# A gated scan and an ELU feed-forward on one core: where the tensors begin in SBUF, shifted to multiples of 512 bytes

## The chip, the cores and the metric

The kernel runs on one core of a Trainium2 chip. The metric is the device time of one launch in microseconds (us). Before the change three runs took 1008.64 us (median), between 1008.42 and 1009.03.

## What is computed

A gated recurrence over 6080 time steps, for 2 sequences of 256 channels, and then a feed-forward layer with an ELU on each of its 12160 outputs:

```python
sig = 1.0 / (1.0 + np.exp(-f_logit))                 # (2, 6080, 256)
f = lower_bound + (1.0 - lower_bound) * sig
for t in range(S):
    h = f[:, t] * h + (1.0 - f[:, t]) * x[:, t]
    y[:, t] = h
u = y.reshape(12160, 256) @ w_in                     # w_in (256, 2048)
g = np.where(u > 0.0, u, np.exp(np.minimum(u, 0.0)) - 1.0)
out = g @ w_out                                      # w_out (2048, 256)
```

## The kernel before, in words

**Layout.** Channels lie on the 128 partitions (256 channels are 2 halves), time runs along the free dimension. A block `j` is 512 steps of both sequences; there are 12 blocks, and the last is 448 steps wide (`width`). The 2048 hidden units are 16 units of 128, taken in 8 pairs `q`.

**Precision.** Every operand of a product is split into a high part of type fp32r and a rest, its low part, of the same type (4 bytes per element each). One product is three matmuls, each with a weight load of 128x128 of its own: high weights by high data, high weights by low data, low weights by high data (`product`, L828 to L837; `second`, L839 to L866). The streamed operand is called the moving one here, the loaded one the weights.

**First product.** For a pair `q` the four tiles C11, C12, C22, C21 (2 units by 2 sequences) are formed out of seven products P1 to P7 in place of eight, from sums of the data (`a_hi`, `a_lo`, `a4_hi`, `a4_lo`) and sums of the weights (`w_in_hi`, `w_in_lo`). They go to PSUM banks `h`; ScalarE copies one bank (`fork`, L434), VectorE makes two additions (`add_u4`, L678; `add_c22`, L686). Block 0 has no summed weights yet and uses plain products (`first_products`, L920 to L942, and `first_product`, L944 to L958), with the low weights in `w_plain_low`.

**ELU.** For each tile ScalarE makes Relu(-h) (L442) and Exp (L448) in `e`, VectorE combines them (L692), ScalarE rounds the result to `g_hi` (L456) and GpSimd subtracts for `g_lo` (L315). `g_hi` and `g_lo` are rings of 8 tiles of 2048 bytes.

**Second product.** For each tile two halves of three matmuls (L860, L861, L862) with moving operand `g_hi`, `g_lo`, `g_hi` add up in PSUM `acc`. They are issued one pair, or two for C21, behind the tile's own products (`whole` of the tensor engine, L868 to L913), so a pair is 45 matmuls: 21 with a moving operand `a...` and 24 with `g...`. A block is 360 matmuls; there are 10 whole blocks of this kind, after block 0 and ahead of the short one.

**Order.** Each engine has its program written out by hand: VectorE's spare work (opening the gates, weighing, the scans, copying `acc` out) stands in fixed places of the pair loop (`spare`, `whole`), and semaphores alone tie the engines. The scan, its loads and the splits of block `j + 1` run in block `j`.

**Memory.** All tensors are allocated one after another in a partition (`sb`, L71); four pairs of names share one room (`alloc_sbuf_tensor_at`). The first free byte at the start, rounded up to 32, is 16512, which is 32 x 512 + 128. All large tensors have a size that is a multiple of 512 bytes. Between `a4_lo` and `e` stand four small ones (`carry`, `bound`, `slope`, `offset`; 16, 8, 8 and 8 bytes, each begun at a multiple of 32), which take 128 bytes in all. A weight operand is 128 columns x 4 bytes = 512 bytes long and begins at its tensor's start plus a multiple of 512; a moving operand is 2048 bytes and begins at its tensor's start plus a multiple of 2048.

```python
        weights_at = -(-nc.sbuf_base // 32) * 32
        sb("weights_room", [P, PAIRS * (in_cols + out_cols) + BATCH * HALVES * TILE])
        nc.tensor.matmul(bank[:, 0:w], hi, a_h[:, 0:w], start=start, stop=False,
        nc.tensor.matmul(bank, hi, g_hi[:, t % RING, 0:w], start=opens, stop=False)
```

Of the kernel before, what the change touches and what calls it, by code (L numbers as in the profile page):

```python
# [8 lines left out]
F32R = mybir.dt.float32r  # L9

P = 128
# [7 lines left out]
TILE = 512  # L19
BLOCKS = -(-SEQ // TILE)  # L20
SHORT = SEQ - (BLOCKS - 1) * TILE
TILES = 4
RING = 8
# [44 lines left out]
def gated_scan_elu_ffn(nc, forget_logit, value, lower_bound, w_in, w_out, out):  # L68
    ctx = ExitStack()
    with ctx:  # L70
        def sb(name, shape, dt=F32):  # L71
            return ctx.enter_context(nc.sbuf_tensor(name, shape, dt))
# [3 lines left out]


        in_cols, out_cols = PRODUCTS * P, 2 * D
        weights_at = -(-nc.sbuf_base // 32) * 32
        sb("weights_room", [P, PAIRS * (in_cols + out_cols) + BATCH * HALVES * TILE])  # L80
        w_in_raw = nc.alloc_sbuf_tensor_at("w_in_raw", [P, PAIRS, PRODUCTS, P], F32, offset=weights_at)
# [21 lines left out]
            w_plain_low.append(nc.alloc_sbuf_tensor_at(f"w_plain_lo{p}", [P, 4, P], F32R, offset=at))  # L103
        a4_hi = sb("a4_hi", [P, TILE], F32R)
        a4_lo = sb("a4_lo", [P, TILE], F32R)
        carry = sb("carry", [P, BATCH, HALVES, 1])
        bound = sb("bound", [P, HALVES])
        slope = sb("slope", [P, HALVES])
        offset = sb("offset", [P, HALVES])

        e = sb("e", [P, TILES, TILE])
        p5 = sb("p5", [P, TILE])
        g_hi = sb("g_hi", [P, RING, TILE], F32R)
        g_lo = sb("g_lo", [P, RING, TILE], F32R)


        h = ctx.enter_context(nc.psum_tensor("h", [P, 4, TILE], F32))
# [894 lines left out]
```

## Time and profile before

| | |
|---|---|
| median of three runs | 1008.64 us |
| the profiled execution | 1008.46 us |
| its span, first to last instruction | 1006.6 us |
| TensorE busy, share of the span | 100% |
| ScalarE, VectorE, GpSimd busy | 79%, 73%, 63% |
| granted TensorE clock | 1.00 of full (2.4 GHz) |

The profile's page gives each engine's busy time, the chain of waits that ended last and the costliest groups of instructions. PE is TensorE's matmul, PEld its weight load, DVE VectorE, ACT ScalarE, POOL GpSimd. A matmul's recorded duration is modelled and overlaps the next one; what a matmul costs in a full stream is the distance between two starts, called its pitch here. Profile times are counted from the span's start. The execution's own time lies 1.86 us over its span.

### The profile page before, as it was taken

Reading aid. Unit: us, or ns where it says so; the run is one execution under the profiler, and the core shown is the slowest. Engines: PE = TensorE matmul, PEld = TensorE weight load, DVE = VectorE, ACT = ScalarE, POOL = GpSimd, SP = SyncE. Lnnn points to the kernel's source line nnn. Section 1 sums busy time; section 2 is a strip of 40 time slices with the busy share of each in tenths; the row PEclk is TensorE's granted clock in tenths of the full one; section 3 lists DMA queues with packets and bytes.
Section 4 is the critical chain, followed back from the end, with each engine's and each line's share of the span. In section 5 each row is a group of like instructions: output and inputs, shape, how many; then the busy total and the mean of one; then the engine's idle time right before and its main releaser. Section 6 shows DMA issues by size and latency. Waiting matters only on the chain.

```text
span 1006.6 us, 15352 instructions
## 1 busy us (share of the span) xinstructions
PE 1001.7 (100%) x4362; PEld 817.3 (81%) x4362; DVE 731.0 (73%) x915; ACT 791.6 (79%) x1425; POOL 631.4 (63%) x474
## 2 busy tenths in 40 slices
PE   9999999999999999999999999999999999999998
PEld 6888888888888888888888888888888888888997
DVE  6995876886786697588679668758867957875544
ACT  7987878777877877877787787787778778778775
POOL 2586887567557557656755855765675575566454
PEclk9999999999999999999999999999999999999999
DMA  7112002101201100210210120011021011000001
GB/s 272 63 32 63 33 1 74 53 1 52 73 0 42 52 31 0 73 52 0 63 63 0 42 63 21 18 55 52 0 64 61 0 46 64 5 0 9 36 1 37
DMA packets 23211, 41.88 MB, mean 42 GB/s; under 512 B 2704, under 2 KB 4240, under 8 KB 23184
## 3 DMA queue, kind: packets, MB, share of 16 engines
q1 hardware_dynamic: 22752, 41.04, 12.6%
q10 hardware_dynamic: 432, 0.53, 0.2%
q8 instruction: 12, 0.20, 0.1%
q14 instruction: 15, 0.12, 0.0%
HBM read 29.10 MB, written 12.45 MB: 41 GB/s over the span
## 4 chain that ended last, share of the span: by engine, by line
PE 99%; DMA 1%; ACT 0%; SPq 0%; DVE 0%; issue 0%
PE acc L862 18%; PE acc L860 18%; PE acc L861 17%; PE h L834 14%; PE h L832 14%; PE h L836 14%; PE h L956 1%; PE h L957 1%; PE h L955 1%; DMA w_in_raw<-w_in 1%; PE h L927 0%; PE h L936 0%; PE acc L927 0%; PE acc L956 0%; PE acc L957 0%; PE acc L955 0%
## 5 line engine op out<-in xcount | busy, mean ns | idle before, releaser
L315 POOL TENSOR_TENSOR g_lo<-e,g_hi 128x512 fp32r<-128x512 f32 (+1 forms) x384 | 518.6, 1359 | 369.5 <-ACT g_hi L456 369.3
L442 ACT ACTIVATE e<-h 128x512 f32<-128x512 f32 (+1 forms) x380 | 225.6, 594 | 166.2 <-PE h L836 135.0
L692 DVE SCALAR_TENSOR_TENSOR e<-e,h 128x512 f32<-128x512 f32 (+1 forms) x380 | 257.1, 677 | 77.3 <-ACT e L448 77.1
L862 PE MATMUL acc<-g_hi,w_out_lo 128*128 128x512 f32 (+1 forms) x768 | 301.9, 393 | 0.0
L860 PE MATMUL acc<-g_hi,w_out_hi 128*128 128x512 f32 (+1 forms) x768 | 301.0, 392 | 0.0
L861 PE MATMUL acc<-g_lo,w_out_hi 128*128 128x512 f32 (+1 forms) x768 | 299.7, 390 | 0.0
L456 ACT CAST g_hi<-e 128x512 fp32r<-128x512 f32 (+1 forms) x384 | 232.2, 605 | 20.7 <-DVE e L692 20.7
L448 ACT ACTIVATE e<-e 128x512 f32<-128x512 f32 (+1 forms) x384 | 241.6, 629 | 8.4
L834 PE MATMUL h<-a_lo,w_in_hi 128*128 128x512 f32 (+1 forms) x616 | 240.8, 391 | 0.0
L832 PE MATMUL h<-a_hi,w_in_hi 128*128 128x512 f32 (+1 forms) x616 | 240.0, 390 | 0.0
L836 PE MATMUL h<-a_hi,w_in_lo 128*128 128x512 f32 (+1 forms) x616 | 238.7, 388 | 0.0
L862 PEld LDWEIGHTS acc<-g_hi,w_out_lo 128*128 128x128 f32 x768 | 144.0, 187 | 32.6
L861 PEld LDWEIGHTS acc<-g_lo,w_out_hi 128*128 128x128 f32 x768 | 144.2, 188 | 31.6
L860 PEld LDWEIGHTS acc<-g_hi,w_out_hi 128*128 128x128 f32 x768 | 144.2, 188 | 30.1
L832 PEld LDWEIGHTS h<-a_hi,w_in_hi 128*128 128x128 f32 x616 | 115.7, 188 | 26.9
L834 PEld LDWEIGHTS h<-a_lo,w_in_hi 128*128 128x128 f32 x616 | 115.6, 188 | 25.0
L836 PEld LDWEIGHTS h<-a_hi,w_in_lo 128*128 128x128 f32 x616 | 115.7, 188 | 24.4
L686 DVE TENSOR_TENSOR h<-p,h 128x512 f32<-128x512 f32 (+1 forms) x88 | 60.5, 687 | 74.5 <-PE h L836 74.5
L601 DVE TENSOR_TENSOR_SCAN x<-gate,carry,x 128x512 f32<-128x512 f32 x48 | 104.2, 2171 | 0.1
L671 DVE COPY p<-h 128x512 f32<-128x512 f32 (+1 forms) x88 | 59.2, 673 | 57.8 <-PE h L836 57.8
L678 DVE TENSOR_TENSOR h<-p,h 128x512 f32<-128x512 f32 (+1 forms) x88 | 60.2, 684 | 39.1 <-PE h L836 38.3
L593 DVE SCALAR_TENSOR_TENSOR x<-gate,x 128x512 f32<-128x512 f32 x48 | 57.3, 1194 | 1.6 <-ACT gate L405 1.3
(72 smaller groups left out, 569.7 us busy)
## 6 DMA issues: line engine op xcount, KB each, us to landing
out<-out_sb SPq DMA_DIRECT2D x44, 256.0 KB, 2.0
gate<-forget_logit SPq DMA_DIRECT2D x43, 256.0 KB, 2.7
x<-value SPq DMA_DIRECT2D x43, 256.0 KB, 2.7
w_in_raw<-w_in SPq DMA_DIRECT2D x8, 256.0 KB, 6.5
w_out_raw<-w_out SPq DMA_DIRECT2D x8, 256.0 KB, 7.4
x<-value SPq DMA_DIRECT2D x4, 224.0 KB, 2.5
gate<-forget_logit SPq DMA_DIRECT2D x4, 224.0 KB, 2.5
out<-out_sb SPq DMA_DIRECT2D x4, 224.0 KB, 2.0
```

The lines of the kernel that those rows point to most:

```text
L315: nc.gpsimd.tensor_tensor(g_lo[:, t % RING, 0:w], e[:, t % TILES, 0:w], g_hi[:, t % RING, 0:w].bitcast(F32), ALU.subtract).then_inc(g_lo_r ...
L442: nc.scalar.activation(e[:, i, 0:w], bank_of(j, t)[:, 0:w], ACT.Relu, scale=-1.0).then_inc(r_ready, 1)
L448: nc.scalar.activation(e[:, t % TILES, 0:w], e[:, t % TILES, 0:w], ACT.Exp, scale=-1.0).then_inc(e_ready, 1)
L456: nc.scalar.copy(g_hi[:, t % RING, 0:w], e[:, t % TILES, 0:w]).then_inc(g_hi_ready, 1)
L601: nc.vector.tensor_tensor_scan(x[:, b, i, 0:w], gate[:, b, i, 0:w], x[:, b, i, 0:w], carry[:, b, i], ALU.mult, ALU.subtract).then_inc(scan ...
L692: nc.vector.scalar_tensor_tensor(e[:, t % TILES, 0:w], e[:, t % TILES, 0:w], -1.0, bank_of(j, t)[:, 0:w], ALU.add, ALU.max).then_inc(g_rea ...
L832: nc.tensor.matmul(bank[:, 0:w], hi, a_h[:, 0:w], start=start, stop=False, skip_group_check=True)
L834: nc.tensor.matmul(bank[:, 0:w], hi, a_l[:, 0:w], start=False, stop=False, skip_group_check=True)
L836: return nc.tensor.matmul(bank[:, 0:w], lo, a_h[:, 0:w], start=False, stop=True, skip_group_check=True)
L860: nc.tensor.matmul(bank, hi, g_hi[:, t % RING, 0:w], start=opens, stop=False)
L861: nc.tensor.matmul(bank, hi, g_lo[:, t % RING, 0:w], start=False, stop=False)
L862: done = nc.tensor.matmul(bank, lo, g_hi[:, t % RING, 0:w], start=False, stop=closes)
```

## The change

Ahead of the weights a tensor `room_before` that nothing reads or writes fills up the space to the next multiple of 512 (384 bytes). The four small tensors move from between `a4_lo` and `e` to the end. No instruction is added, removed or reordered on any engine; the addresses in them are all that differs.

```diff
@@ -76,6 +76,9 @@
         in_cols, out_cols = PRODUCTS * P, 2 * D
+
+        base = -(-nc.sbuf_base // 32) * 32
+        sb("room_before", [P, -base % 512], mybir.dt.uint8)
         weights_at = -(-nc.sbuf_base // 32) * 32
         sb("weights_room", [P, PAIRS * (in_cols + out_cols) + BATCH * HALVES * TILE])
@@ -103,15 +106,14 @@
         a4_hi = sb("a4_hi", [P, TILE], F32R)
         a4_lo = sb("a4_lo", [P, TILE], F32R)
+        e = sb("e", [P, TILES, TILE])
+        p5 = sb("p5", [P, TILE])
+        g_hi = sb("g_hi", [P, RING, TILE], F32R)
+        g_lo = sb("g_lo", [P, RING, TILE], F32R)
         carry = sb("carry", [P, BATCH, HALVES, 1])
         bound = sb("bound", [P, HALVES])
         slope = sb("slope", [P, HALVES])
         offset = sb("offset", [P, HALVES])
-
-        e = sb("e", [P, TILES, TILE])
-        p5 = sb("p5", [P, TILE])
-        g_hi = sb("g_hi", [P, RING, TILE], F32R)
-        g_lo = sb("g_lo", [P, RING, TILE], F32R)
```

The starts, in bytes of a partition, and what is left of them over a multiple of 512, as the allocations give them:

| tensor | before | over 512 | after | over 512 |
|---|---|---|---|---|
| `w_in_raw`, `w_in_lo` | 16512 | 128 | 16896 | 0 |
| `w_out_raw`, `w_out_lo` | 45184 | 128 | 45568 | 0 |
| `out_sb`, `w_plain_lo0` to `3` | 61568 | 128 | 61952 | 0 |
| `w_in_hi` | 69760 | 128 | 70144 | 0 |
| `w_out_hi` | 98432 | 128 | 98816 | 0 |
| `gate`, `x` | 114816, 123008 | 128 | 115200, 123392 | 0 |
| `a_hi`, `a_lo` | 131200, 155776 | 128 | 131584, 156160 | 0 |
| `a4_hi`, `a4_lo` | 180352, 182400 | 128 | 180736, 182784 | 0 |
| `e`, `p5` | 184576, 192768 | 256 | 184832, 193024 | 0 |
| `g_hi`, `g_lo` | 194816, 211200 | 256 | 195072, 211456 | 0 |
| `carry` and the other three | 184448 to 184552 | | 227840 to 227944 | |

So before, weights and `a...` lie 128 bytes over a multiple of 512, and `e`, `p5` and `g...` 256 bytes over one.

## Rows read from the trace of the kernel before

**Rows 1.** The page: span, and busy time of each engine

```profile
span 1006.6 us, 15352 instructions
...
PE 1001.7 (100%) x4362; PEld 817.3 (81%) x4362; DVE 731.0 (73%) x915; ACT 791.6 (79%) x1425; POOL 631.4 (63%) x474
```

**Rows 2.** The waits, TensorE alone: who for whom, us in total, times, longest

```profile
PE h L963 <- POOL e L372: 1.3, 1, 1.3
PE h L927 <- ACT a_hi L417: 0.5, 1, 0.5
```

**Rows 3.** Stretches, TensorE alone, one whole block each: length, busy time (count), clock

```profile
340.31:423.55 83.24, 83.24 (x362) 1.00 0.12 38
506.79:590.03 83.24, 83.24 (x362) 1.00 0.12 38
```

**Rows 4.** Timeline of TensorE in block 0: start us, us, instruction

```profile
11.80 0.39 PE L933 MATMUL h<-a_lo,w_in_hi 128*128 128x512 f32 x1
...
17.25 0.39 PE L955 MATMUL h<-a_hi,w_in_hi 128*128 128x512 f32 x1
...
18.61 0.40 PE L860 MATMUL acc<-g_hi,w_out_hi 128*128 128x512 f32 x1
...
20.00 0.39 PE L955 MATMUL h<-a_hi,w_in_hi 128*128 128x512 f32 x1
...
21.38 0.40 PE L860 MATMUL acc<-g_hi,w_out_hi 128*128 128x512 f32 x1
```

**Rows 5.** Timeline of TensorE in a whole block, around its third pair

```profile
451.98 0.40 PE L860 MATMUL acc<-g_hi,w_out_hi 128*128 128x512 f32 x1
452.21 0.39 PE L861 MATMUL acc<-g_lo,w_out_hi 128*128 128x512 f32 x1
452.43 0.40 PE L862 MATMUL acc<-g_hi,w_out_lo 128*128 128x512 f32 x1
452.67 0.39 PE L860 MATMUL acc<-g_hi,w_out_hi 128*128 128x512 f32 x1
452.90 0.40 PE L861 MATMUL acc<-g_lo,w_out_hi 128*128 128x512 f32 x1
453.14 0.39 PE L862 MATMUL acc<-g_hi,w_out_lo 128*128 128x512 f32 x1
...
454.07 0.39 PE L832 MATMUL h<-a_hi,w_in_hi 128*128 128x512 f32 x1
```

**Rows 6.** Timeline of TensorE at the end of its warm-up, bf16 matmuls on `e`

```profile
7.07 1.03 PE L963 MATMUL h<-e 128*128 128x512 bf16 x4
...
7.50 0.59 PE L963 MATMUL h<-e 128*128 128x512 bf16 x2
```

**Rows 7.** Timeline of TensorE in the last block, 448 columns wide

```profile
984.37 0.36 PE L832 MATMUL h<-a_hi,w_in_hi 128*128 128x448 f32 x1
...
985.60 0.36 PE L860 MATMUL acc<-g_hi,w_out_hi 128*128 128x448 f32 x1
...
1000.06 0.36 PE L862 MATMUL acc<-g_hi,w_out_lo 128*128 128x448 f32 x1
...
1002.91 0.37 PE L861 MATMUL acc<-g_lo,w_out_hi 128*128 128x448 f32 x1
```

**Rows 8.** Timeline of VectorE up to the addition that P4 of rows 5 waits for

```profile
441.87 0.70 DVE L686 TENSOR_TENSOR h<-p,h 128x512 f32<-128x512 f32 x1 [0.47 <-PE h L836]
...
443.89 0.69 DVE L692 SCALAR_TENSOR_TENSOR e<-e,h 128x512 f32<-128x512 f32 x1 [0.74 <-ACT e L448]
444.50 2.32 DVE L601 TENSOR_TENSOR_SCAN x<-gate,carry,x 128x512 f32<-128x512 f32 x1
...
450.00 1.79 DVE L593 SCALAR_TENSOR_TENSOR x<-gate,x 128x512 f32<-128x512 f32 x1
451.71 1.52 DVE L586 TENSOR_SCALAR gate<-gate,slope,offset 128x512 f32<-128x512 f32 x1
453.15 0.68 DVE L686 TENSOR_TENSOR h<-p,h 128x512 f32<-128x512 f32 x1
```

**Rows 9.** Groups of instructions on ScalarE: busy, mean ns of one, idle before

```profile
L456 ACT CAST g_hi<-e 128x512 fp32r<-128x512 f32 (+1 forms) x384 | 232.2, 605 | 20.7 <-DVE e L692 20.7
...
L427 ACT CAST a_hi<-x 128x512 fp32r<-128x512 f32 (+1 forms) x33 | 20.4, 617 | 0.0
```

**Rows 10.** The chain of waits in order of time, its beginning: start us, us, what

```profile
1.65 5.74 DMA w_in_raw<-w_in
7.41 0.62 ACT w_in_hi L464
8.03 0.53 ACT a_hi L417
8.60 1.25 PE h L927 x4
```

## The prediction

> **What bounds the kernel now.** Read the page's busy times first [rows 1]: TensorE is busy for 1001.7 of 1006.6 us. That alone doesn't say that it works at its best, since a matmul's end is modelled, so the second view is its waits [rows 2]: 1.3 us for its first operand and 0.5 us before the first real product, and nothing after. From 8.6 us to the end TensorE never waits for anyone. The third view is the stretches [rows 3]: two whole blocks far apart take 83.24 us each for 360 matmuls (the two more in the count reach over an edge), 231.2 ns a matmul. The clock is granted in full, so 512 columns at 2.4 GHz would be 213.3 ns, and 17.9 ns of each pitch is something else. It repeats to the hundredth of a microsecond from block to block, while the other engines' work around it differs. So the kernel is a row of 4362 pitches, and the question is what an address does to a pitch.
>
> The timeline answers part of it. In block 0, from 11.80 to 18.61 us, 30 matmuls have a moving operand `a...` only [rows 4]: 6.81 / 30 = 227.0 ns each. Then groups of six with `g...` alternate with six with `a...`: 18.61 to 20.00 is 1.39 us, 20.00 to 21.38 is 1.38 us, so 231.7 and 230.0 ns. In a whole block's run of nine with `g...` the distances go 0.23, 0.22, 0.24, 0.23, 0.24 and so on [rows 5], and 454.07 - 451.98 = 2.09 us is 232.2 ns each; leave out the first two and it is 1.64 / 7 = 234 ns. So with `g...` as moving operand a matmul comes to cost about 7 ns more than with `a...`, and the first few `a...` after a run of `g...` still pay part of it, which is why the mean is 231.2 and not the mean of 227 and 234 over the kinds alone.
>
> What differs between the two kinds? Not the columns, the type, the weight's size or the order high, low, high. Not PSUM: in the stretch of 30 the banks of both `h` and `acc` are written (`FIRST_BANK`), and they average the 227 all the same. Not which weight: their starts step by 512 bytes, and the pitch follows neither high nor low; it alternates by two where the operands change by three [rows 5]. What is left is that `a...` begins 128 bytes over a multiple of 512, as the weights do, and `g...` 256 over one, or 128 bytes apart from the weights. Since the load of the next weights runs beside the streaming of the present operand, and the pitch alternates and has an aftermath, I take it that the two reads of TensorE meet each other in SBUF, and that their distance within 512 bytes sets how often. After the change this distance is 0 everywhere, as it is for `a...` now.
>
> **The change part by part.**
>
> *The distance between `g...` and the weights goes from 128 to 0 bytes.* Every 512-column matmul then has the pitch of the stretch of 30. I use 226.7 ns, 0.3 under the quotient of those rows, as they include the tail of a start-up; either value is within their rounding (6.81 us to a hundredth, over 30). A whole block becomes 360 x 0.2267 = 81.61 us in place of 83.24, saving 1.63; ten of them save 16.3 us. Block 0 has 25 periods of twelve matmuls, each 2.77 us now [rows 4] and 12 x 0.2267 = 2.72 after: 25 x 0.05 = 1.2 us; its last 12 matmuls with `g...` give 12 x 0.007 = 0.1 us. In the last block the pitch is 2.85 / 14 = 203.6 ns with `g...` and 1.23 / 6 = 205 ns with `a...` [rows 7], alike, so I take nothing there but for the 30 matmuls of the block before it that lag into it: 0.15 us. Sum: 16.3 + 1.2 + 0.1 + 0.15 = 17.75 us.
>
> *The common offset goes from 128 to 0.* The trace has no operand at 0. By my reading only the distance counts and this is worth nothing. The bounds from rows: at best the matmul falls to the 216 ns of the warmed-up bf16 matmuls (four take 1.03 us and the last two of them 0.59, so a pitch is 0.44 / 2 = 0.22, a little under in finer time) [rows 6], at worst it goes to 234 ns. I take 226.7, since that row is nearest in everything but the common offset; the ends are rivals below.
>
> *What is late next.* With TensorE 1.9% faster, the place with least room is in the third pair of each block: VectorE works without a pause from 444.50 to 453.83 us [rows 8] (the end of its addition at L686, 453.15 + 0.68), and TensorE's P4 at 454.07 waits for that addition [rows 5]. The room is 0.24 us. VectorE's run begins behind an Exp (443.89) that hangs on the same addition one pair earlier, which started at 441.87 as soon as TensorE let it [rows 8]. From there to this P4 are 12.2 us, 53 matmuls, so TensorE will come earlier by 53 x 4.5 ns = 0.24 us, the whole room. With a semaphore's way P4 then waits about 0.05 us, once a block: 0.5 us in all. Behind the waiting matmul stands all of TensorE's queue, so this is on the path. If VectorE's operations were faster through the alignment there would be nothing; if its shared work with GpSimd fell worse by 0.1 us, another 1 us. I take 0.5, with 0 and 1.5 as ends.
>
> *The other engines' operands.* ScalarE's rounding takes 605 ns from `e` to `g_hi`, both 256 over, and 617 ns from `x` to `a_hi`, both 128 over [rows 9], means that mix some narrow tiles in. So these engines hardly see the offset; 2% either way, hidden behind TensorE. At the start the first weights' transfer of 5.74 us leads to the first product [rows 10]. Its rows of 2048 bytes now land on multiples of 512. Nothing in the trace shows a price; a tenth of the transfer, 0.6 us, either way bounds it. I take 0.
>
> *The four small tensors and the padding.* No one waits for where they lie, and the padding isn't touched: nothing.
>
> The sum goes against the profiled execution's 1008.46 us, 0.18 under the median: 1008.46 - 17.75 + 0.5 = 991.2. This case's own range is 988.5 to 993.5.
>
> A rule speaks against all of this. The Trainium skill, "SBUF — State Buffer", section "Who interferes with whom", gives TensorE two read ports, one for the moving operand and one for the weight load, and calls them independent. By that rule addresses would not matter and the sum would be 0. The trace doesn't settle it in words, but two kinds of matmul with different pitches under the same clock and the same shape are hard to fit to it. The page "TensorE: Matmul & The Clock Gate", section "Back-to-back issue gap", gives N / 2.4 + 2.5 ns for a warm matmul, 216 for 512 columns; the warm-up agrees [rows 6], the fp32r matmuls here do not.
>
> **The rivals.**
>
> *Aligned reads are cheaper still.* If a 512-byte weight that begins on a multiple of 512 spares something that one across a boundary pays, all pitches fall below 226.7. For it: 256 over costs more than 128 over, which continued gives about 220 at 0. Against: the alternation and the aftermath point at a meeting of two reads, not at a fee per boundary. Price: to the floor of 216 a block takes 77.8 us, 5.4 less; with block 0 about 59 us. P4's wait then grows to 53 x 15 ns - 0.24 = 0.6 us a block, 6 us in all, so 1008.5 - 59 + 6 = 955. Halfway, at 221, it is 1008.5 - 39 + 3 = 972. I write 965 for it.
>
> *The address isn't the cause.* `g...` is also the operand that ScalarE and GpSimd have just written and lies high in memory. Then nothing moves: 1008.5 us. For it: no pair of rows differs in the address alone. Against: the first matmuls of a run of `a...` after `g...` pay too, and whole blocks repeat to 0.01 us [rows 3] though the writers' timing within them varies. The two-port rule of the Trainium skill's page "SBUF — State Buffer" would lead to this case.
>
> *The common offset counts, the wrong way (the other side).* An operand at 0 might meet the load at its worst, since both reads then begin on the same boundary at once. The price is 234 ns for every matmul: a block takes 84.2 us, 1.0 more; with block 0 about 11.5 us, so 1020. It decides the sign as soon as the pitch at 0 is over 231.2 ns. For it: no row is at 0. Against: `a...` and the weights have the same offset already, and that is the cheaper kind.
>
> **How the numbers follow.** Chances: my forecast 0.55, cheaper still 0.20, no change 0.14, slower 0.11. A difference under 0.2%, 2 us, is about what a measurement of this kernel can't tell from none. So faster 0.75, same 0.14, slower 0.11. The range goes up to the case of no change, 1009, and leaves out the slower one; down it goes to 962, which leaves out the outer third of the cheaper case: 0.55 + 0.13 + 0.14 = 0.82 inside.
>
> **What would show it.** Right: whole blocks of 81.6 to 81.7 us in the stretches, all 512-column pitches at 226 to 227 with no alternation in a run of `g...`, the last block's 203.6 ns unchanged, and at most some small waits of TensorE for L686. Wrong: a pitch for `a...` off 227 (then the common offset counts), or `g...` still at 234 (then the address isn't the cause). If TensorE shows waits of more than 2 us in all, the gain is right and the cover was thinner than I read it.

## The result and the profile after

The changed kernel took 991.78 us (median of four runs, 991.58 to 992.14) against 1008.53 us of the kernel before beside it: a ratio of 0.9833, 95% interval 0.9816 to 0.9851. The forecast was 991.2 us. The profiled execution has a span of 989.8 us, 16.8 less than [rows 1].

The page's busy times and TensorE's waits:

```profile
span 989.8 us, 15352 instructions
PE 983.3 (99%) x4362; PEld 816.4 (82%) x4362; DVE 727.9 (74%) x915; ACT 791.4 (80%) x1425; POOL 631.7 (64%) x474
```

```profile
PE h L929 <- ACT a_hi L419: 1.3, 1, 1.3
PE h L965 <- POOL e L374: 1.3, 1, 1.3
PE h L957 <- issue: 0.6, 1, 0.6
```

The other engines do the same work in the same time to within 0.5%; their share rises only because the span is shorter. All of the difference is TensorE's. Its waits have a new row of 0.6 us, to which we come below. The wait ahead of the first product is 1.3 us where it was 0.5 [rows 2], but it costs nothing: the warm-up ended earlier in this execution, and the product itself began at 8.23 us in place of 8.60. Lines of the code lie two further down than before.

Here are two stretches of TensorE's, each from the start of P4 in the third pair of a block to the same start one block later, against 83.24 us in [rows 3]. TensorE is busy throughout, so the length between two such starts is what there is to read, here and in the stretches below, which run from a block's first matmul to the next block's:

```profile
283.18:364.86 81.68, 81.68 (x362) 1.00 0.12 39
446.54:528.22 81.68, 81.68 (x361) 1.00 0.12 39
```

TensorE's timeline in block 0 and at the third pair of a whole block, against [rows 4, 5]:

```profile
18.39 0.39 PE L862 MATMUL acc<-g_hi,w_out_hi 128*128 128x512 f32 x1
...
19.75 0.39 PE L957 MATMUL h<-a_hi,w_in_hi 128*128 128x512 f32 x1
...
21.11 0.39 PE L862 MATMUL acc<-g_hi,w_out_hi 128*128 128x512 f32 x1
```

```profile
444.50 0.39 PE L862 MATMUL acc<-g_hi,w_out_hi 128*128 128x512 f32 x1
444.73 0.39 PE L863 MATMUL acc<-g_lo,w_out_hi 128*128 128x512 f32 x1
444.95 0.39 PE L864 MATMUL acc<-g_hi,w_out_lo 128*128 128x512 f32 x1
...
446.54 0.45 PE L834 MATMUL h<-a_hi,w_in_hi 128*128 128x512 f32 x1
446.82 0.40 PE L836 MATMUL h<-a_lo,w_in_hi 128*128 128x512 f32 x1
```

Six matmuls with `g...` take 1.36 us and six with `a...` take 1.36 us: 226.7 ns each, where [rows 4] had 1.39 and 1.38. The run of nine takes 446.54 - 444.50 = 2.04 us, 226.7 ns each, where [rows 5] had 2.09, and the distances no longer alternate. Between the first two matmuls of P4, though, lie 0.28 us in place of 0.23. The addition that P4 waits for ends just ahead of it:

```profile
444.32 1.52 DVE L588 TENSOR_SCALAR gate<-gate,slope,offset 128x512 f32<-128x512 f32 x1
445.75 0.68 DVE L688 TENSOR_TENSOR h<-p,h 128x512 f32<-128x512 f32 x1
```

It ends at 446.43, 0.11 us before the recorded start of P4, where the room was 0.24 us before ([rows 8]). In nine of the ten whole blocks this distance is 0.28 to 0.29 us, and those blocks take 81.68 us; the first has none of it and takes 81.60, which is 360 x 226.67 ns.

The 0.6 us gap is in block 0. TensorE, and VectorE's ELU just before it:

```profile
76.64 0.39 PE L864 MATMUL acc<-g_hi,w_out_lo 128*128 128x512 f32 x1
77.64 0.47 PE L957 MATMUL h<-a_hi,w_in_hi 128*128 128x512 f32 x1 [0.61 <-issue]
```

```profile
76.85 0.69 DVE L694 SCALAR_TENSOR_TENSOR e<-e,h 128x512 f32<-128x512 f32 x1 [0.68 <-ACT e L450]
```

The matmul that starts at 77.64 belongs to tile 28. By `FIRST_BANK` it goes to bank 3, which tile 26 used last, and the ELU at 76.85 is tile 26's; it ends at 77.54. The "issue" of the trace is this wait for a PSUM bank. It costs 1.00 - 0.23 = 0.77 us, and the next distance is 0.08 longer too: 0.85 us in all.

### The profile page after: what moved, and what is told of

Its sections match the earlier page's. It is cut to its first block, busy times and chain, and to the rows that moved or that the text cites. A ratio compares the mean times of both kernels' runs of the same rounds, so it can differ in the third digit from the quotient of the medians.

```text
span 989.8 us, 15352 instructions
## 1 busy us (share of the span) xinstructions
PE 983.3 (99%) x4362; PEld 816.4 (82%) x4362; DVE 727.9 (74%) x915; ACT 791.4 (80%) x1425; POOL 631.7 (64%) x474
## 4 chain that ended last, share of the span: by engine, by line
PE 99%; DMA 1%; DVE 0%; issue 0%; ACTq 0%; ACT 0%
PE acc L864 17%; PE acc L862 17%; PE acc L863 17%; PE h L834 14%; PE h L836 14%; PE h L838 14%; PE h L957 1%; PE h L959 1%; PE h L958 1%; DMA x<-value 1%; PE h L938 0%; DVE x L603 0%; PE h L929 0%; PE acc L959 0%; PE acc L957 0%; PE acc L938 0%
## 5 line engine op out<-in xcount | busy, mean ns | idle before, releaser
L864 PE MATMUL acc<-g_hi,w_out_lo 128*128 128x512 f32 (+1 forms) x768 | 297.3, 387 | 0.0
L862 PE MATMUL acc<-g_hi,w_out_hi 128*128 128x512 f32 (+1 forms) x768 | 297.3, 387 | 0.0
L836 PE MATMUL h<-a_lo,w_in_hi 128*128 128x512 f32 (+1 forms) x616 | 238.4, 387 | 0.0
```

What stands on the lines that cost most here:

```text
L836: nc.tensor.matmul(bank[:, 0:w], hi, a_l[:, 0:w], start=False, stop=False, skip_group_check=True)
L864: done = nc.tensor.matmul(bank, lo, g_hi[:, t % RING, 0:w], start=False, stop=closes)
```

## The experiments

All times are medians beside runs of the kernel before on the same chip (1008.6 to 1008.8 us).

### Which part of the change does it

The change does two things: it moves everything to a multiple of 512, and it brings `e`, `p5` and `g...` to the same offset as the weights. These three runs take them apart.

Only the small tensors moved (the padding left out of the changed kernel):

```diff
-        base = -(-nc.sbuf_base // 32) * 32
-        sb("room_before", [P, -base % 512], mybir.dt.uint8)
```

> Only the four small tensors move to the end; no padding ahead of the weights, so weights, data and g all begin 128 bytes over a multiple of 512. Theory (the distance between the moving operand and the weights within 512 bytes sets the pitch): distance 0 everywhere as in the changed kernel, 991.8 us within 1 us, all 512-column pitches 226.7 ns. Rival (a start at a multiple of 512 is what is cheap): no better than the a... operands before, also 226.7 ns; if g... at 128 costs less or more than a..., the difference shows in its rows.

Measured: 992.12 us, ratio 0.9835 (0.9819 to 0.9852). Half of the diff, and none of the alignment, gives all of the gain.

Only the padding (the other half of the diff, the small tensors where they were):

```diff
+        base = -(-nc.sbuf_base // 32) * 32
+        sb("room_before", [P, -base % 512], mybir.dt.uint8)
         weights_at = -(-nc.sbuf_base // 32) * 32
```

> Only the padding ahead of the weights; the small tensors stay in the middle, so weights and a... begin at 0 and e, p5 and g... at 128 over a multiple of 512. Theory of the distance: as before the change, since g... is again 128 past the weights: 1008.5 us within 1.5, g pitches alternating 229 and 238 ns. Rival (the moving operand's own start over 512 counts: 128 is cheap, 256 dear, 0 at least as cheap): 991.8 us, all pitches 226.7 ns.

Measured: 1008.28 us, ratio 0.9996 (0.9987 to 1.0006): no difference from before. The weights and `a...` are at a multiple of 512 here, and the whole gain is missing. `g...` begins at 128 over a multiple, as `a...` did before the change at 227 ns, and costs what it cost at 256 over.

All at 256 over a multiple of 512:

```diff
-        sb("room_before", [P, -base % 512], mybir.dt.uint8)
+        sb("room_before", [P, (256 - base) % 512], mybir.dt.uint8)
```

> The changed kernel with all starts 256 bytes over a multiple of 512, padding and all. Theory of the distance: 991.8 us within 1 us, nothing changes. Rival (a moving operand that begins at 256 over is dear, whatever the weights do): every 512-column pitch goes to 234 ns, a block to 84.2 us, the kernel to about 1020 us.

Measured: 992.0 us, ratio 0.9835 (0.9818 to 0.9851). The offset that `g...` had when it was dear is cheap once the weights have it as well.

A whole block of each (the small tensors alone, the padding alone, all at 256), by the stretches:

```profile
335.58:417.27 81.69, 81.69 (x361) 1.00 0.12 39
```

```profile
340.41:423.64 83.23, 83.23 (x361) 1.00 0.12 38
```

```profile
335.04:416.73 81.69, 81.69 (x361) 1.00 0.12 39
```

So the moving operand's own start does not count, and neither does the common one. The distance between the two operands does.

### The price of each distance

Here TensorE runs extra stretches of 24 matmuls behind its last product, with no other computation beside most of them. They write PSUM banks that nothing reads any more. `CASES` gives the weights' start, the moving operand's start (in elements of 4 bytes) and the columns:

```diff
+CASES = ([(w, m, 512) for w in (0, 32, 64, 96) for m in (0, 32, 64, 96)]
+         + [(0, m, 512) for m in (1, 2, 4, 8, 16, 24, 40, 48, 80, 112)]
+         + [(16, 16, 512), (8, 16, 512)]
+         + [(0, 0, n) for n in (480, 448, 384, 256)] + [(0, 32, n) for n in (480, 448, 384, 256)])
...
+                weights = w_in_hi[:, :, :, :].rearrange("p a b c -> p (a b c)")[:, w_at:w_at + P]
+                moving = a_hi[:, :, :, :].rearrange("p a b c -> p (a b c)")[:, m_at:m_at + columns]
+                for k in range(24):
...
+                        nc.tensor.matmul(bank, weights, moving, start=k % 3 == 0, stop=k % 3 == 2)
```

> The changed kernel, and behind its last product 34 stretches of 24 matmuls that only write unused PSUM banks: weights at 0, 128, 256, 384 past a multiple of 512 by the moving operand at 0, 128, 256, 384 (16 stretches of 512 columns); weights at 0 with the moving operand at 4, 8, 16, 32, 64, 96, 160, 192, 320 and 448 bytes; both at 64; weights at 32 and moving at 64; then 480, 448, 384 and 256 columns, with the moving operand at 0 and again at 128. 34 x 24 x 0.23 = 180 us more or so in all. Theory of the distance: the four stretches with equal starts cost 226.7 ns each, the four with the moving operand 128 past the weights 233.4, and the other distances are constant along a diagonal too. Rival of the moving start: the price follows the moving operand's start alone. Rival of a fee per boundary crossed: only weights at 0 are cheapest. By width: if the weight load sets a floor, 448 and fewer columns stay near 203 ns.

TensorE's timeline, the rows for weights at 0 and then at 128 with the moving operand at 0, 128, 256, 384, and behind "..." weights at 0 with the moving operand at 4, 8, 16, 32 and 64 bytes (start us, us, instruction; two lines of code in turn, so that each stretch has its own row):

```profile
987.63 5.63 PE L997 MATMUL h<-a_hi,w_in_hi 128*128 128x512 f32 x24
993.09 5.75 PE L995 MATMUL h<-a_hi,w_in_hi 128*128 128x512 f32 x24
998.68 5.62 PE L997 MATMUL h<-a_hi,w_in_hi 128*128 128x512 f32 x24
1004.14 5.75 PE L995 MATMUL h<-a_hi,w_in_hi 128*128 128x512 f32 x24
1009.73 5.76 PE L997 MATMUL h<-a_hi,w_in_hi 128*128 128x512 f32 x24
1015.33 5.62 PE L995 MATMUL h<-a_hi,w_in_hi 128*128 128x512 f32 x24
1020.78 5.75 PE L997 MATMUL h<-a_hi,w_in_hi 128*128 128x512 f32 x24
1026.37 5.62 PE L995 MATMUL h<-a_hi,w_in_hi 128*128 128x512 f32 x24
...
1076.02 5.85 PE L997 MATMUL h<-a_hi,w_in_hi 128*128 128x512 f32 x24
1081.70 5.77 PE L995 MATMUL h<-a_hi,w_in_hi 128*128 128x512 f32 x24
1087.31 5.72 PE L997 MATMUL h<-a_hi,w_in_hi 128*128 128x512 f32 x24
1092.87 5.76 PE L995 MATMUL h<-a_hi,w_in_hi 128*128 128x512 f32 x24
1098.47 5.66 PE L997 MATMUL h<-a_hi,w_in_hi 128*128 128x512 f32 x24
```

Read the distance between starts over 24, or, leaving the first three of a stretch out, from the fourth start to the last over 20, as in this table:

| distance in bytes, moving less weights | pitch, ns |
|---|---|
| 0 (four offsets) | 226.7, the first stretch 227.2 |
| 0 (both operands at 64) | 227.8 |
| 256 (four) | 226.65 |
| 128 (four), 384 (four) | 233.3 |
| 64, 320 | 228.75 |
| 16 | 231.65 |
| 8, 32 (weights at 0, and at 32), 192, 448 | 233.3 |
| 96, 160 | 234.0, 234.35 |
| 4 | 236.7 |

The sixteen of the grid fall into two prices, strictly by distance, so the rival of the moving start and the fee per boundary both fall: weights at 128, 256 and 384 have a multiple of 512 inside them, weights at 0 have none, and at the same distance they cost the same. The 227.8 ns of the stretch with both operands at 64 is a slow beginning: its first nine matmul distances average 232 ns and the others 226.6; other stretches begin slowly too, for three to five matmuls. I had not expected that 0 and 256, and 128 and 384, are alike: the pattern repeats after 256 bytes, not 512. With 512 columns none of the distances tried is cheaper than 0. Fewer columns give no clear rule: with the operands 0 and 128 apart 480 columns take 216.7 and 217.65 ns, 448 take 206.4 and 203.55, 384 take 173.3 and 175.45, 256 take 119.7 and 118.7. So with 448 and 256 columns the distance of 128 is the cheaper one in these stretches. Nor do the stretches of 448 carry over to the kernel: in the last block of the changed kernel, with the distance 0 throughout, the 448-column matmuls take 202.6 ns on average and not 206.4. Why is open. A floor of 203 ns from the weight load, which the last block's nearly equal pitches [rows 7] suggested, does not exist, since 384 columns take 173.3.

### Does the price carry back into the kernel

A dear distance for every product, and a cheap one by another number. Both kernels leave room behind the weights, 32 bytes in one and 256 in the other:

```diff
+APART = 32
...
+        sb("apart", [P, APART], mybir.dt.uint8)
         gate = sb("gate", [P, BATCH, HALVES, TILE])
```

> The changed kernel with 32 bytes left free between the weights and everything behind them: every moving operand is then 32 bytes past the weights within 512 (233.35 ns in the probe, the same as 128). Theory: 6.7 ns more for each of the 360 matmuls, blocks of 84.0 in place of 81.68 us, block 0 about 2 us more less the 0.85 us wait that it has now, so 1015.5 us (1013 to 1018), slower than before the change. Rival (only multiples of 128 or 512 bytes matter, or the probe does not carry over to the kernel): 992 or 1008 us.

> The same with 256 bytes left free: weights at 0 and all data at 256 over a multiple of 512. Theory of a distance that repeats after 256 bytes, as the probe showed: 991.8 us within 1. Rival (it repeats after 512, the probe's stretches without other engines' work do not carry over): above 1000 us.

Measured with 32 bytes: 1018.05 us, ratio 1.0092 (1.0076 to 1.0107). With 256 bytes: 992.0 us, ratio 0.9835 (0.982 to 0.985). A whole block of each:

```profile
343.47:427.47 84.00, 84.00 (x362) 1.00 0.12 37
```

```profile
334.84:416.52 81.68, 81.68 (x362) 1.00 0.13 39
```

84.00 us is what 360 x 233.35 ns gives. The total is 2.5 us over my estimate and just outside its range of 1013 to 1018. 1.5 us of that is the last, short block, which I had taken as unchanged: its 448-column matmuls go from a mean of 203 ns to 207. Thirty-two bytes of empty room are worth 26 us here, and the kernel before the change lay between the two since only its `g...` had a bad distance.

### How the two reads meet

The last question is why. Narrower weights shorten the load, and bf16 halves the bytes of both operands.

```diff
+CASES = ([(0, m, n) for n in (128, 96, 64, 32) for m in (0, 32)]
+         + [(0, m, 128) for m in (3, 5, 6, 12, 14, 20, 28, 36, 44, 52, 56, 60, 63, 65)])
...
+                nc.tensor.matmul(h[:, k % 4, :], zeros[:, 0:P], zeros[:, 64:64 + TILE], start=True, stop=True)
...
+                weights, moving = weights[:, w_at:w_at + w_columns], moving[:, m_at:m_at + TILE]
```

> The changed kernel with stretches of 24 matmuls that only write unused PSUM banks. Three stand right behind the bf16 warm-up and read its zeros: weights at 0, moving operand at 128, 256 and 4 bytes. The others stand behind the last product, fp32r, 512 columns: weights of 128, 96, 64 and 32 columns, each with the moving operand at 0 and at 128 bytes; then weights of 128 columns with the moving operand at 12, 20, 24, 48, 56, 80, 112, 144, 176, 208, 224, 240, 252 and 260 bytes. Theory (the load's reads meet the stream's reads, and the distance sets how often): the surcharge over 213.3 ns shrinks with the number of weight columns, at 128 bytes from 20 ns towards 5 at 32 columns, at 0 bytes from 13.3 towards 3; bf16, half the bytes of both, pays little at any distance. Rival (each matmul has a fixed fee by its type and the moving operand's place, the load has no part in it): the pitch is the same for 32 and for 128 weight columns. 12 to 252 bytes: between 226.7 and 237 all, and 260 like 4 (236.7), since distances repeat after 256.

The timeline: bf16 with the moving operand at 128, 256 and 4 bytes, then fp32r with weights of 96, 64 and 32 columns, each at 0 and at 128 bytes; and the weight load's own rows (busy us, mean ns):

```profile
6.89 5.34 PE L970 MATMUL h<-e 128*128 128x512 bf16 x24
12.07 5.34 PE L972 MATMUL h<-e 128*128 128x512 bf16 x24
17.25 5.34 PE L974 MATMUL h<-e 128*128 128x512 bf16 x24
```

```profile
1011.14 5.71 PE L1002 MATMUL h<-a_hi,w_in_hi 128*96 128x512 f32 x24
1016.68 5.71 PE L1000 MATMUL h<-a_hi,w_in_hi 128*96 128x512 f32 x24
1022.23 5.68 PE L1002 MATMUL h<-a_hi,w_in_hi 128*64 128x512 f32 x24
1027.76 5.72 PE L1000 MATMUL h<-a_hi,w_in_hi 128*64 128x512 f32 x24
1033.31 5.71 PE L1002 MATMUL h<-a_hi,w_in_hi 128*32 128x512 f32 x24
1038.86 5.69 PE L1000 MATMUL h<-a_hi,w_in_hi 128*32 128x512 f32 x24
```

```profile
L1000 PEld LDWEIGHTS h<-a_hi,w_in_hi 128*128 128x128 f32 x24 | 4.5, 188 | 1.1
...
L1000 PEld LDWEIGHTS h<-a_hi,w_in_hi 128*32 128x32 f32 x24 | 2.6, 108 | 2.9
```

bf16 takes 215.8 ns at each of the three distances, as expected. The fp32r part went against me: the load shrinks from 188 to 108 ns, but the pitch does not fall. It is 230.2 and 231.65 ns with 96 weight columns (distance 0 and 128), 229.75 and 231.25 with 64, 231.35 and 230.65 with 32, where 128 columns give 226.7 (227.2 in this run, with its slow beginning) and 233.35. The rival of a fee without any part of the load falls as well, as the width does change the pitch, up at distance 0 and down at 128. With the finer steps (12 bytes 228.9, 20 236.0, 24 233.4, 48 and 56 230.0, 80 231.2, 112 231.15, 144 233.35, 176 231.0, 208 234.65, 224 233.35, 240 and 252 226.7, 260 236.65) the repetition after 256 bytes holds again: 260 is like 4. That the surcharge depends on how the two operands lie to each other is shown; that it comes from their reads meeting in SBUF, more of them the longer the load, is not. Why the best distance still takes 226.7 ns, 11 more than bf16, stays open as well. A matmul without its load was not tried, and in no run did a matmul's own weights lie otherwise than those loaded for the next one, so which of the two counts is not told apart.

### The two waits that the faster TensorE ran into

Tile 28 of block 0 to a bank that has been free longer:

```diff
-              + [3, 2, 3, 1])
+              + [1, 2, 3, 1])
```

> The changed kernel with one entry of the table of PSUM banks in block 0 other: the tile 28 goes to bank 1, last used by tile 24, and not to bank 3, last used by tile 26, whose ELU ends 0.1 us before TensorE's first matmul of tile 28. Theory (the 0.6 us gap in the changed kernel at 77.03 us is the wait for that bank): the gap goes, block 0 is 0.85 us shorter, 990.9 us. Rival (TensorE waits there for something else, weights or the data's low part): the gap stays, 991.8 us.

Measured: 991.35 us, ratio 0.9828 (0.9815 to 0.9842). The gap is gone, from the row of waits too, and the stretch of block 0 from the first matmul with `g...` to the end went from 71.59 to 70.72 us, 0.87 less. Its median is 0.4 to 0.95 us below the changed kernel's own (991.78, and 992.3 below). The medians alone would not show the gain, since the program's opening differs by as much: the first matmul with `g...` starts between 18.33 and 19.13 us in the traces of the kernels at distance 0.

And VectorE's gate opening behind its addition instead of ahead of it:

```diff
                     weigh(n, 0, 1)
-                    open_gate(n, 1, 0)
...
+                if at == (2, 3):
+                    open_gate(n, 1, 0)
...
                     elu(j, t + C12)
+                    spare(j, par, q, 3, last)
                     elu(j, t + C22)
```

> The kernel of the run with the other bank, and besides VectorE opens gate (1, 0) of the next block not ahead of its addition for C22 in the third pair, but between the ELUs of C12 and C22, where it has 0.7 us of idle time. Theory (TensorE's P4 in the third pair waits for that addition, which stands behind this work): the 0.08 us by which nine of ten whole blocks are longer than 360 x 226.67 ns goes, 0.72 us in all, so 0.7 us under that run's 991.35, 990.6 us, every whole block 81.60 us. Rival (the wait is for PSUM or data written by another engine): blocks stay at 81.68. If the ELU of C22 now comes late, the copy that the next pair's P2 waits for does too, and blocks grow.

> The changed kernel once more, beside the one before, as the measure for the small differences of e8 and e9: 991.8 us within 0.4, blocks of 81.68 us, a gap of some 0.8 us in block 0.

Measured: 990.62 us for the two edits, ratio 0.9821 (0.9808 to 0.9835), and 992.3 us for the changed kernel once more, ratio 0.9841 (0.9827 to 0.9854). A whole block of each:

```profile
333.88:415.48 81.60, 81.60 (x361) 1.00 0.12 39
```

```profile
335.51:417.19 81.68, 81.68 (x361) 1.00 0.12 39
```

VectorE in the third pair with both edits:

```profile
441.46 1.79 DVE L595 SCALAR_TENSOR_TENSOR x<-gate,x 128x512 f32<-128x512 f32 x1
443.66 0.70 DVE L688 TENSOR_TENSOR h<-p,h 128x512 f32<-128x512 f32 x1 [0.40 <-PE h L840]
444.26 0.68 DVE L694 SCALAR_TENSOR_TENSOR e<-e,h 128x512 f32<-128x512 f32 x1
444.86 0.54 DVE L588 TENSOR_SCALAR gate<-gate,slope,offset 128x512 f32<-128x512 f32 x1
```

The addition now waits for TensorE (0.40 us) and not TensorE for it, and the gate opening, 1.52 us long in its old place, takes 0.54 in its new one. What it ran beside differs, GpSimd's subtraction for `g_lo`. Here is first the changed kernel's in the old place. Then come, with both edits, the two around the new place, and the one beside the block's next gate opening with that gate opening itself:

```profile
443.80 1.75 POOL L317 TENSOR_TENSOR g_lo<-e,g_hi 128x512 fp32r<-128x512 f32 x1
```

```profile
442.67 1.74 POOL L317 TENSOR_TENSOR g_lo<-e,g_hi 128x512 fp32r<-128x512 f32 x1
446.24 1.30 POOL L317 TENSOR_TENSOR g_lo<-e,g_hi 128x512 fp32r<-128x512 f32 x1 [1.83 <-ACT g_hi L458]
...
451.61 1.29 POOL L317 TENSOR_TENSOR g_lo<-e,g_hi 128x512 fp32r<-128x512 f32 x1 [1.58 <-ACT g_hi L458]
451.70 1.48 DVE L588 TENSOR_SCALAR gate<-gate,slope,offset 128x512 f32<-128x512 f32 x1
```

In the old place the subtraction ends at 445.55 us and the gate opening at 445.84. In the new place, from 444.86 to 445.40, no subtraction runs. The next gate opening of the block took 0.82 us in the changed kernel; it now has nearly a whole subtraction beside it and takes 1.48. Every whole block is 81.60 us. This is the best version of the study, 1.7 us below the changed kernel in the same set of runs.

## Why the prediction was right

**The step that carries the sum**, that the distance between `g...` and the weights goes to that of `a...` and the weights, and that the pitch is then 226.7 ns everywhere, held to the tenth of a nanosecond for 512 columns. The inference behind it, from a before that had no row at the new addresses, was tested against its nearest rivals by the runs with half of the diff each and with all starts at 256. Both halves of the inference stand: the distance counts and the common start does not.

**Term by term.** Whole blocks: forecast 16.3 less 0.5 for the new wait, 15.8 us; measured 10 x (83.24 - 81.68) and 0.08 for the first, 15.7 us. The wait itself: forecast 0.05 us a block, for which no row was given, measured 0.08 in nine blocks, with P4 starting 0.11 us behind the end of the addition. (VectorE's run ahead of it was not quite without a pause, as I had read it: the trace before has 0.10 us of one ahead of 448.70. It changes nothing in the sum.) Block 0: forecast 1.3 us; the pitches gave 1.24 (71.96 us before from the first matmul with `g...` to the end of the block, 70.72 in the run with the other bank), but a second cover gave way that I had not looked for and took 0.87 of it back, at tile 28. The program's opening, which I had put at nothing, was 0.22 us shorter in the profiled execution, less than it differs by from run to run. Last block and end: forecast 0.15 us, measured 0.53, since the 448-column matmuls, which I had taken as unchanged, went from a mean of 203.8 ns to 202.6. The missed wait and the two small gains partly cancel, so 991.2 against 991.8 owes a little to luck.

**The cover I missed.** I took block 0 as 25 periods of a faster TensorE and looked for thin covers in the whole blocks alone. In block 0 the ELU chain of ScalarE and VectorE runs at its own pace: tile 26's ELU starts 58.46 us behind the first matmul with `g...` in both traces (76.85 less 18.39, and 77.07 less 18.61), while TensorE would have come to tile 28 after 58.48 us (76.87) where it took 59.49 before (78.10).

**The rivals.** "The address isn't the cause" fell with the result and with the 32 bytes that cost 26 us. "The common offset counts" fell by the runs with the small tensors alone (all at 128) and with all at 256, as fast as the one at 0. "Aligned reads are cheaper still" fell with the grid of stretches: weights on a multiple of 512 cost as much as weights across one. The Trainium skill's statement of two independent read ports ("SBUF — State Buffer", "Who interferes with whom") fits the bf16 stretches here, 215.8 ns at all three distances. For fp32r it does not hold in its effect: the pitch goes from 226.7 to 236.7 ns with nothing changed but the distance of the two operands. The Trainium skill's page "TensorE: Matmul & The Clock Gate", "Back-to-back issue gap", gives its 216 ns for 512 columns as the gap of a matmul by itself; here it agrees with the bf16 stretches, 215.8 ns, and not with fp32r.

**The mechanism.** Only its outside was right. My reading that the load's reads and the stream's reads meet would have the surcharge shrink with the load, and it did not.

## What to carry to other kernels

When TensorE never waits, measure the pitch of its matmuls by operand: two kinds of the same shape with different pitches are a gain to be had, here 1.7% for moving 128 bytes of small tensors. With fp32r operands and 512 columns keep the weights' and the moving operand's starts a multiple of 256 bytes apart; which multiple, and where they begin in themselves, made no difference here. For fewer columns measure it: with 448 and 256 a distance of 128 bytes was a little cheaper in the stretches. After any such gain look for work that had just been in time, in the opening block as well as in the steady ones: here two such places were worth 1.7 us.

## What the runs showed of the hardware that I had not expected

- An fp32r matmul of 512 columns at the full clock takes between 226.65 and 236.7 ns by the distance of its operands in SBUF, in a pattern that repeats after 256 bytes where that was tried (4 and 260 bytes: 236.7 and 236.65; 0, 240, 252 and 256: 226.7).
- Fewer weight columns shorten the load (188, 161, 134 and 108 ns for 128, 96, 64 and 32) and do not shorten the pitch: at distance 0 it rises from 226.7 to 231.35 ns.
- The same VectorE operation (opening a gate, 512 columns) took 1.52 us in its old place of the loop and 0.54 behind the next ELU in the same pair. Its length goes with GpSimd's subtraction for `g_lo`: of the 420 gate openings in the ten traces without extra stretches, 401 began beside a running subtraction, and 390 of these ended 0.28 to 0.29 us behind its end, up to 1.53 us long; the other 11 began near its end and took 0.54. With none beside, it took 0.53 to 0.54 us, 19 times. Why is not shown.
